# Row maxima by single chunk and bank, one copy of sums and values per head, and a division on gathered sums

## The reference

```python
q_pool = q.reshape(B, H, S // 2, 2, D).mean(axis=3)          # S = 1152, D = 64: 576 query rows
scores = (1 / sqrt(D)) * np.matmul(q_pool, k.transpose(0, 1, 3, 2))   # 576 x 1152
scores = scores - np.max(scores, axis=-1, keepdims=True)
attn = np.exp(scores)
attn = attn / (np.sum(attn, axis=-1, keepdims=True) + 1e-09)
x = np.matmul(attn, v)                                        # 576 x 64 of each head
h = x @ w_in;  x = (h * tanh(softplus(h))) @ w_out            # 1152 tokens, 512 -> 2048 -> 512
h = x @ w_in2; x = where(h > 0, h, exp(min(h, 0)) - 1) @ w_out2
```

## Time and profile before

| | |
|---|---|
| time, median of 3 runs | 705.26 us (703.49 to 706.42) |
| the profiled execution | 703.71 us, its span 701.9 us |
| PE busy, share of the span | 657.8 us, 94% |
| POOL, DVE, ACT busy | 426.5, 423.4, 397.0 us |
| waits of PE for the reduction of maxima | 14.9 us in 32 waits |

### The profile page before, as it was taken

The page is one execution under the profiler, slowest core; times in us unless marked ns, Lnnn a source line. Parts: engine busy times, 40 slices in busy tenths (PEclk is TensorE's granted clock), DMA queues, the critical chain, the costliest instruction groups (busy, mean ns, idle before and its releaser), DMA issues.

```text
span 701.9 us, 12236 instructions
## 1 busy us (share of the span) xinstructions
PE 657.8 (94%) x3984; PEld 636.7 (91%) x3984; DVE 423.4 (60%) x620; ACT 397.0 (57%) x743; POOL 426.5 (61%) x388
## 2 busy tenths in 40 slices
PE   3589999999999999999999999999999999999997
PEld 2478889898898988899999999999999999999997
DVE  6667878787887876377777665777543332223222
ACT  2357888888888878755555555555643322222221
POOL 4266788888888866587786666787644422222221
PEclk9599999999999999999999999999999999999999
DMA  5355564555556540012220000122222110001001
GB/s 162 96 155 157 147 174 135 163 159 158 143 147 163 157 110 16 16 50 71 62 61 0 0 0 30 48 67 67 60 77 61 46 45 0 0 0 46 1 1 45
DMA packets 31503, 54.30 MB, mean 77 GB/s; under 512 B 4752, under 2 KB 10208, under 8 KB 31456
## 3 DMA queue, kind: packets, MB, share of 16 engines
q1 hardware_dynamic: 31296, 53.66, 27.7%
q10 hardware_dynamic: 160, 0.04, 0.0%
HBM read 30.93 MB, written 2.36 MB: 47 GB/s over the span
## 4 chain that ended last, share of the span: by engine, by line
PE 67%; POOL 8%; ACT 8%; DVE 7%; issue 7%; DMA 2%; SPq 1%; POOLq 0%; ACTq 0%; DVEq 0%
PE py L490 9%; PE py L491 8%; PE py L492 8%; PE pH L475 8%; PE pH L476 8%; PE pH L477 8%; PE pm L398 5%; DVE part_max L712 3%; PE po L430 3%; PE po L431 3%; PE po L432 3%; PE ps L413 3%; PE ps L414 3%; POOL pl L931 3%; ACT ph L565 2%
## 5 line engine op out<-in xcount | busy, mean ns | idle before, releaser
L986 POOL TENSOR_TENSOR gl<-fg,gh 128x384 fp32r<-128x384 f32 x96 | 97.3, 1014 | 142.4 <-ACT gh L655 141.1
L931 POOL TENSOR_TENSOR pl<-p,ph 128x576 fp32r<-128x576 f32 x72 | 106.0, 1480 | 67.4 <-ACT p L571 63.3
L712 DVE TENSOR_REDUCE part_max<-pm 128x2 f32<-128x768 f32 (+1 forms) x123 | 111.1, 904 | 39.9 <-PE pm L398 38.1
L490 PE MATMUL py<-gh,wout_h 128*128 128x384 f32 x384 | 129.2, 336 | 3.6 <-DVE xl L842 2.2
L491 PE MATMUL py<-gl,wout_h 128*128 128x384 f32 x384 | 128.4, 334 | 0.0
L492 PE MATMUL py<-gh,wout_l 128*128 128x384 f32 x384 | 128.3, 334 | 0.0
L477 PE MATMUL pH<-xh,win_l 128*128 (+1 forms) x384 | 128.3, 334 | 0.0
L475 PE MATMUL pH<-xh,win_h 128*128 (+1 forms) x384 | 128.3, 334 | 0.0
L476 PE MATMUL pH<-xl,win_h 128*128 (+1 forms) x384 | 128.3, 334 | 0.0
L565 ACT ACTIVATE ph<-ps 128x576 fp32r<-128x576 f32 x144 | 93.9, 652 | 51.2 <-PE ps L414 48.8
L821 DVE RECIPROCAL fi<-fp 128x192 f32<-128x192 f32 x48 | 64.9, 1353 | 52.2 <-POOL fp L994 52.1
(11 more groups left out here) (68 smaller groups left out, 1367.7 us busy)
## 6 DMA issues: line engine op xcount, KB each, us to landing
kh<-k_hi SPq DMA_DIRECT2D x60, 144.0 KB, 2.6
w_raw<-w_in SPq DMA_DIRECT2D x32, 256.0 KB, 2.7
w_raw<-w_out SPq DMA_DIRECT2D x32, 256.0 KB, 2.6
k_pack<-kP SPq DMA_DIRECT2D x16, 288.0 KB, 3.2
q_raw<-qT SPq DMA_DIRECT2D x16, 288.0 KB, 3.1
v_raw<-v SPq DMA_DIRECT2D x16, 288.0 KB, 2.9
kl<-k_pack SPq DMA_DIRECT2D x32, 144.0 KB, 2.4
q<-q SPq DMA_DIRECT2D x16, 144.0 KB, 2.5
```

The source lines that it names most:

```text
L490: pe.matmul(out, hi, gh[:, f % 4, :], start=(f == 0), stop=False)
L712: dve.tensor_reduce(part_max[:, par, 2 * g:2 * g + wide], group_banks(n, g)[:, 0:wide, 0:MC], AX.X, ALU.max).then_inc(m_read, 1)
L931: pool.tensor_tensor(pl[:, ph_slot(slot, kt), :], p32[:, p32_slot(n, kt) % 3, :], ph[:, ph_slot(slot, kt), :].bitcast(F32), ALU.subtract). ...
```

## The change

1. **Maxima.** From head 1 on, a chunk of 384 columns goes to one of the banks `pm` alone, and is reduced alone: 15 reductions a head in place of 8, and PE fills one bank while DVE reads the other. Head 0 keeps its groups. Four chunks of head 1 come before the first scores.
2. **Copy.** One copy a head of all 128 rows of `po` into `o_rows`, at the first step of the next head instead of two copies of 64 rows at the last step.
3. **Division.** `gather_sums` moves a row of 576 sums of each head to 64 x 9 elements; DVE adds 1e-9 and inverts 128 x 9; `gather_inv` brings each half back as one row of `inv_wide`, and `spread_inv` copies that row to 63 partitions; `move_o` brings the odd head's values to the lower partitions; `finalize` is one multiplication. `scale_by_partner`, `multiply_sums`, `copy_sum` are gone. These transfers are all issued on SP's queue, as `spread_row` now is too.
4. **Order.** `pv` always follows the scores of its step; `POOL_KT` alternates; the splits of k, q, v, w and x move to other steps; DVE's stream is written by chunk. SP's order is new.

```diff
-POOL_KT = ((2, 4, 5, 6, 8), (2, 4, 5, 8))
+POOL_KT = ((1, 3, 5, 7, 8), (1, 3, 5, 7))
...
-FIRST_GROUPS = (2, 2, 2, 2, 0, 1, 1, 1, 2)
-GROUPS = (1, 1, 1, 0, 1, 1, 1, 1, 1)
-
-
-GPSIMD_AT = {"split_v": (0, 0), "multiply_sums": (1, None), "sum_q": (3, 3), "split_w": (4, 4),
-             "split_k": (6, 6), "split_q": (7, 7), "split_x": (None, 7)}
-SCALAR_AT = {"split_v": (0, 0), "split_w": (2, 2), "spread_row": (4, 4), "round_k": (4, 4), "split_q": (5, 5),
-             "split_x": (None, 5)}
-VECTOR_AT = {"scale": (1, None), "invert_0": (3, None), "invert_1": (5, None), "finalize": (None, 3)}
+
+EARLY_CHUNKS = 4
+FIRST_CHUNKS = ((2, 1), (2, 1), (2, 2), (1, 0), (1, 1), (1, 1), (1, 1), (1, 1), (1, 1))
+CHUNKS = ((1, 0), (2, 0), (2, 0), (0, 0), (2, 0), (1, 1), (2, 0), (1, 1), (1, 1))
+
+
+FIRST_SPLIT_BEHIND = {3: (1, 0), 6: (1, 2), 10: (1, 4), 14: (1, 6)}
+SPLIT_BEHIND = {3: (2, 8), 5: (1, 0), 8: (1, 2), 12: (1, 4), 14: (1, 6)}
+INVERT_BEHIND, FINALIZE_BEHIND = 14, 6
+
+
+GPSIMD_AT = {'split_k': (0, 0), 'sum_q': (3, 2), 'split_v': (3, 1), 'split_q': (8, 4), 'split_w': (5, 7), 'split_x': (0, None)}
+SCALAR_AT = {'split_v': (0, 0), 'split_w': (1, 2), 'round_k': (3, 5), 'split_q': (7, 6), 'split_x': (None, 7)}
...
+            def gather_sums(m):
+                par, pair = m % 2, m // 2
+                sp.wait_ge(o_copied, m + 1)
+                wait(sp, sum_kept, pair)
+                source = D * (1 - par)
+                sp.dma_start(sum_few[par * D:par * D + D, :],
+                             o_rows[source:source + 1, par, :].rearrange("o (r c) -> o r c", c=FEW)).then_inc(sums_in[par], 16)
+
+            def move_o(p):
+                sp.wait_ge(o_copied, 2 * (p + 1))
+                sp.wait_ge(sums_in[0], 16 * (p + 1))
+                sp.dma_start(o_rows[D:2 * D, 0, :], o_rows[D:2 * D, 1, :]).then_inc(o_moved, 16)
+
+            def gather_inv(p):
+                sp.wait_ge(sum_inv, p + 1)
+                wait(sp, x_ready, p)
+                for par in range(2):
+                    sp.dma_start(inv_wide[par * D:par * D + 1, :].rearrange("o (r c) -> o r c", c=FEW),
+                                 inv_few[par * D:par * D + D, :]).then_inc(inv_in, 16)
+
+            def spread_inv(p):
+                sp.wait_ge(inv_in, 32 * (p + 1))
+                for par in range(2):
+                    first = par * D
+                    sp.dma_start(inv_wide[first + 1:first + D, :],
+                                 inv_wide[first:first + 1, :].unsqueeze(1).to_broadcast([1, D - 1, SQ])).then_inc(inv_spread, 16)
...
             next_q(1)
             spread_kl(0)
             spread_q2(0)
+            spread_row(0)
             next_q(2)
             spread_kh(1)
             spread_q1(1)
...
             for n in range(HEADS):
-                if n + 2 < HEADS:
-                    load_v(n + 2)
                 if n + 1 < HEADS:
                     load_w(w_in[0][n + 1], 0, n + 1, (n + 1) % 2)
+                if n % 2 == 0 and n > 0:
+                    gather_sums(n - 1)
+                    move_o(n // 2 - 1)
+                elif n % 2:
+                    gather_sums(n - 1)
+                if n + 1 < HEADS:
+                    spread_row(n + 1)
+                if n % 2 == 0 and n > 0:
+                    gather_inv(n // 2 - 1)
                 if n + 2 < HEADS:
                     spread_kl(n + 2)
                     spread_q2(n + 2)
+                if n % 2 == 0 and n > 0:
+                    spread_inv(n // 2 - 1)
+                if n + 2 < HEADS:
+                    load_v(n + 2)
                 if n + 3 < HEADS:
                     spread_kh(n + 3)
                     spread_q1(n + 3)
                 if n + 4 < HEADS:
                     next_q(n + 4)
                     load_kp(n + 4)
+            gather_sums(HEADS - 1)
+            move_o(PAIRS - 1)
+            gather_inv(PAIRS - 1)
+            spread_inv(PAIRS - 1)
...
+            def max_chunk(n, j):
+
+                at, (t, c) = chunk_count(n, j), divmod(j, 3)
+                if j == 0:
                     pe.wait_ge(kh_spread, 64 * (n + 1))
                     pe.wait_ge(q1_spread, 64 * (n + 1))
-                wait(pe, m_read, NG * n + g - (2 if n == 0 else 0))
-                for j in range(2 * g, min(2 * g + 2, NCH)):
-                    t, c = divmod(j, 3)
-                    mm = pe.matmul(group_banks(n, g)[:, j % 2, 0:MC], q1[:, n % 3, t * P:t * P + P],
-                                   kh[n % 3][:, c * MC:c * MC + MC], start=True, stop=True)
-                mm.then_inc(m_filled, 1)
+                wait(pe, m_read, at - 1)
+                pe.matmul(pm[:, at % 2, 0:MC], q1[:, n % 3, t * P:t * P + P], kh[n % 3][:, c * MC:c * MC + MC],
+                          start=True, stop=True).then_inc(m_filled, 1)
...
+            for j in range(EARLY_CHUNKS):
+                max_chunk(1, j)
...
                     nxt = ahead(n, kt)
-                    if kt + AHEAD < KT:
+                    if nxt is not None:
                         scores(*nxt)
-                        for head, g in groups_at(n, kt):
-                            max_group(head, g)
-                        pv(n, kt)
-                    else:
-                        pv(n, kt)
-                        if nxt is not None:
-                            scores(*nxt)
-                        for head, g in groups_at(n, kt):
-                            max_group(head, g)
+                    for head, j in chunks_at(n, kt, 0):
+                        max_chunk(head, j)
+                    pv(n, kt)
+                    for head, j in chunks_at(n, kt, 1):
+                        max_chunk(head, j)
...
-                wait(act, x_scaled, n // 2)
-                own = slice(n % 2 * D, n % 2 * D + D)
-                act.activation(halves(o_pair[own, :]), po[own, :, 0:HQ], ACT.Copy).then_inc(o_copied, 1)
-
-            def copy_sum(n):
-
-                wait(act, sum_prod, n // 2)
-                own, other = slice(n % 2 * D, n % 2 * D + D), slice(D - n % 2 * D, 2 * D - n % 2 * D)
-                act.activation(halves(sum_pair[own, :]), po[other, :, 0:HQ], ACT.Copy, bias=1e-9).then_inc(sum_copied, 1)
+                if n % 2 == 0:
+                    wait(act, x_ready, n // 2)
+                else:
+                    wait(act, o_moved, 16 * (n // 2))
+                    wait(act, sums_in[1], 16 * (n // 2))
+                act.activation(halves(o_rows[:, n % 2, :]), po[:, :, 0:HQ], ACT.Copy).then_inc(o_copied, 1)
...
+            def max_chunk(n, j):
+                at, par = chunk_count(n, j), n % 2
+                dve.wait_ge(m_filled, at + 1)
+                dve.tensor_reduce(part_max[:, par, j:j + 1], pm[:, at % 2, 0:MC], AX.X, ALU.max).then_inc(m_read, 1)
+                if j == NCH - 1:
+                    dve.wait_ge(m_read, at + 1)
+                    turn_row(n)
...
+            def invert(p):
+
+                dve.wait_ge(sums_in[0], 16 * (p + 1))
+                dve.wait_ge(sums_in[1], 16 * (p + 1))
+                dve.tensor_scalar(sum_few[:, :], sum_few[:, :], 1e-9, None, ALU.add).then_inc(sum_kept, 1)
+                dve.wait_ge(sum_kept, p + 1)
+                wait(dve, inv_in, 32 * p)
+                dve.reciprocal(inv_few[:, :], sum_few[:, :]).then_inc(sum_inv, 1)
...
+            def finalize(p):
+                dve.wait_ge(inv_spread, 32 * (p + 1))
+                dve.wait_ge(o_moved, 16 * (p + 1))
                 wait(dve, xl_done, p)
-                dve.tensor_tensor(halves(x_pair[:, :]), halves(o_pair[:, :]), halves(sum_pair[:, :])[:, ::-1, :],
-                                  ALU.mult).then_inc(x_scaled, 1)
-
-            def finalize(p):
-                dve.wait_ge(sum_inv, 2 * (p + 1))
-                dve.wait_ge(x_scaled, p + 1)
-                dve.tensor_tensor(halves(x_pair[:, :]), halves(x_pair[:, :]),
-                                  inv_pair[:, :].unsqueeze(1).to_broadcast([P, 2, HQ]),
-                                  ALU.mult).then_inc(x_ready, 1)
+                dve.tensor_tensor(x_pair[:, :], o_rows[:, 0, :], inv_wide[:, :], ALU.mult).then_inc(x_ready, 1)
...
+            for m in range(1, HEADS + 2):
+                for j in range(NCH):
+                    if m < HEADS:
+                        max_chunk(m, j)
+                    if j == INVERT_BEHIND and m % 2 and 3 <= m < HEADS:
+                        invert((m - 3) // 2)
+                    if j == FINALIZE_BEHIND and m % 2 == 0 and 4 <= m <= HEADS:
+                        finalize((m - 4) // 2)
+                    if j in (SPLIT_BEHIND if m > 1 else FIRST_SPLIT_BEHIND):
+                        back, kt = (SPLIT_BEHIND if m > 1 else FIRST_SPLIT_BEHIND)[j]
+                        if 0 <= m - back < HEADS and kt in VKT[(m - back) % 2]:
+                            split_p(m - back, kt)
+
+            invert(PAIRS - 1)
```

(62 more changed lines are left out.)

105 lines of the change are left out of this document (51 added, 54 removed).

## The result

| | before | after |
|---|---|---|
| time, median | 705.15 us (703.49 to 706.42) | 775.37 us (773.92 to 776.05) |
| the profiled execution | 703.71 us, span 701.9 | 776.05 us, span 774.1 |
| mean granted clock of PE | 0.987 | 0.933 |

What follows compares the result with a forecast made beforehand. PE was taken as the bound, with a gap of about a tenth in attention. Pairs -13.0, start +2.3, end of attention -1, into the network +6.6 sum to -5.1: 700.2 us against the median of 705.26, range 690 to 709.

Steps and rivals of the forecast that it cites:

- Its landing is the unknown ... I take 3.0: Division: spread_inv lands 3.0 us after its last issue begins, so PE loses 1.0 us a pair with the restart.
- The broadcast lands late: Division, rival at 0.20: both spread_inv read one partition and land at 3.9 us instead of 3.0; 705 us.
- the count of engines: Division: by the Trainium skill's rule the broadcast's 63 partitions go to 9 DMA engines, making the late landing likelier.
- What the clock took: Start of the network: PE's clock falls in a 5.8 us gap and costs +2 us (0 to +5.8).
- The chunks: Maxima in attention: PE's 2.35 us a pair of waits for the reduction go, if DVE is not held.
- One copy and splits: Attention pairs: the single copy costs 0.3 us in one head of two; 0.23 us a pair stays for splits.
- The start: Head 0: moves queued behind spread_row delay first scores to about 30.3 us; step 5 comes +2.3 us (0 to +5).
- The end of attention: Last heads: no chunks, alternating tiles, the last one DVE's; -1 us (-2 to +1).
- Into the network: From attention to the first network: the division's transfers and finalize delay multiply_h by 4.6 us, +6.6 with the clock.
- The SP rival: SP's queue, rival at 0.17: 39 issues a pair become the bound, from 0.73 us an issue; 712 us.
- Seven pairs: Attention, step 5 of head 0 to head 14: 1.85 us less a pair, -13.0 us in all.

Runs made afterwards that it cites:

- the mended kernel: Changed kernel with the inverse through HBM, start, end and SP order moved, no 1e-9 addition, last product one chunk earlier: 690.22 us, ratio 0.9797.

## Why the prediction was wrong

**The step that failed** is one number: "Its landing is the unknown ... I take 3.0". What leads up to it came out within a microsecond. Counted from step 0 of the even head, where the prediction's t begins (its scores start at 110.41 in the pair shown), the last scores of the head began at 8.8 (8.2 counted), `spread_kl` was issued at 9.7 (8.9), the last `spread_inv` at 12.3 (11.3), and DVE stood ready for `finalize` at 13.9 (13.15). The inverse was to be there at 14.3 and came at 23.1. The landing was not 3.0 but 10.8 us. With that number alone the prediction's own sum gives a stall of 0.9 + 7.8 = 8.7 a pair; measured 8.6 here, and 8.5 in the mean of six pairs.

**Why 3.0 was taken.** Of the rows that it lay between the earlier trace rows one reads 64 partitions and the other HBM (`k_pack<-kP`); the broadcast reads one partition. The text said so ("no row shows such a read"), and yet bounded the unknown by 2.0 and 3.9. That was no bound from rows, since none of them showed the case. A range without an upper row had to be left open upward, and the forecast with it, since the order of SP's queue puts DVE and PE behind this landing.

**The rival that named the place** was priced wrong. "The broadcast lands late" had the mechanism, one source partition, and put its size at 0.9 us, for which it showed no row. The runs part it from the count of engines, the rule that stood beside it: 63 rows instead of 64 cost 1.8 us where each row has its own partition and at most 0.6 where all come from one; the single partition costs 7.8 (11.0 against 3.2). In the Trainium skill, "SBUF — State Buffer", section "Door 1: The DMA port swizzle (why `[64,N]` ≈ `[32,N]`)", four neighbouring partitions share one port of about 27 GB/s. An estimate by that page for one transfer of 145 KB is 5.4 us of reading. The run has 8.6 us for one transfer alone, 1.8 of which is the median landing of `gather_inv`'s 2.2 KB: 6.8 for the rest, and the page is borne out in kind. By that estimate a landing is 7.2 us, 4.2 later than taken, in seven pairs and at the end: a rival at about 734.

**What the clock took.** It was counted at the end (+2) but not in a pair, since a gap of 1 us was forecast there. The gap of 8.2 to 8.6 brought it down in each of the six pairs, and with it 2.1 us in the mean. So a pair of 41.3 instead of 30.55 is, roughly, 7.5 us of longer stall, 2.1 of clock, 0.8 of the splits below, and 0.4 of `invert`'s wait. Only six of the seven pairs have a division beside them; the sum took the stall for all seven.

**The chunks.** "The 2.35 us go, if DVE is not held" held only in the new order: with chunks alone 0.1 of it came in six pairs. In the mended kernel the profile shows no idle time of PE ahead of `pm` in pairs of 30.4. So the term is right in the whole, and wrong as a part.

**One copy and splits** were under-sized together, and mistaken in kind. 0.3 + 0.23 a pair were counted. In a mended pair of 30.4 the first `pv` of each head starts 0.45 us late, but what ends that wait is DVE's split of tile 0 (done at 82.71, PE at 82.74); the copy was done at 82.48, so it cost nothing by itself. The other 0.2 in each head stand behind the two chunks in a row at step 6, where the second waits for its bank. That is 1.3 in all:

```profile
82.74 0.37 PE L496 MATMUL po<-ph,vt 128*128 128x288 f32 x1 [0.21 <-DVE pl L790]
```

That is why a pair without any stall is 30.4 (30.41 measured; 29.0 + 1.3 is 30.3) and not 29.5.

**Two terms were left out.** `invert` can wait for its gathered sums, ahead of a split: up to 1.5 us a pair. The sums' 2.2 KB were taken to land in 2.1 us; in the changed kernel they took 3.3 in the median and 4.3 at most. And DVE's small operations were taken at the length of work without a neighbour, 0.4 for addition and inversion together and 0.8 for the product; beside GpSimd the addition took up to 1.46 and the product up to 1.98.

**The start** was right in kind: first scores at 29.95 (30.3 counted), step 5 of head 0 at +0.9 instead of +2.3, inside its bounds. **The end of attention** was to gain 1; it lost 7.8, since the copy of head 14 waits for the product of the pair before, and PE for that copy (8.3). **Into the network** the chain was counted right but for the same landing: from the first issue of `gather_inv` to that of `spread_inv` 3.1 us (2.7 counted), then 11.1 to `finalize` instead of 3.3:

```profile
356.79 1.16 SPq L370 DMA_DIRECT2D inv_wide<-inv_few  x2
359.93 1.60 SPq L377 DMA_DIRECT2D inv_wide<-inv_wide  x2
```

```profile
370.99 0.76 DVE L806 TENSOR_TENSOR x_pair<-o_rows,inv_wide 128x576 f32<-128x576 f32 x1 [14.23 <-DMA inv_wide<-inv_wide]
```

**The SP rival** (712) did not come: 1.59 us for two issues of the broadcast, 0.8 each, but the queue's lateness followed the broadcast and wasn't its cause, since without it the pair is 31.2 with all other issues in place.

**Slips of the sums**, none of which moves the forecast: by the earlier trace rows DVE's reductions before come to 13.1 us a pair, not 13.4; the case of the late broadcast adds up to +2.1, not +2.3; and at the start the clock came back 11.6 us after PE resumed, not 11.7.

**The rest of the idea was sound.** Seven pairs were to gain 13.0 us; in the mended kernel (690.22 us) they gain 11.75 (215.7 against 227.5), the start 1.5, the end of attention 1.3, the way into the network 0.4, and the network loses 0.4: 14.5 of span.

## What to carry to other kernels

Before a transfer is priced by its bytes, ask from how many partitions it reads and by what its row count divides: here the time out of one source partition grew with the rows, and a row in HBM, or a source of 64 partitions, brought 11 us down to 3 to 5. An unknown that stands ahead of other work in an in-order queue is not one term of a sum; it can grow without cover, so measure it first or put what waits for it last. And when a wait is removed, ask which engine has no gap around that place: with chunks alone the gain stayed out, by my reading (no run shows it) for ACT's and POOL's backlog.

## What the runs showed of the hardware

- Two transfers, each from one partition, are not independent: one alone 8.6 us, two from partitions 0 and 64 11.0, two from the same one 12.8. In the Trainium skill, "SBUF — State Buffer", section "Door 1: The DMA port swizzle (why `[64,N]` ≈ `[32,N]`)", partitions 0 and 64 lie on different ports; what they share here stays open.
- 61 rows of 2304 bytes, each from its own partition, two transfers: 16.1 us; 64 rows: 3.2.
- DVE's addition on 128 x 9 elements took 0.17 to 1.46 us and its product of two SBUF tensors 0.76 to 1.98, by what GpSimd was doing; its reciprocal of one tensor (0.20 to 0.22) and its splits, which read PSUM (0.71 to 0.76), kept their length. The Trainium skill, "SBUF — State Buffer", section "🔬 SBUF: two separate sides", has an exclusive lock of the port pair that a DVE operation with two SBUF inputs, or in a 2-port mode, shares with GpSimd; the trace agrees, with 110.80 and 204.90 as the two orders.
- In the six long gaps of the changed kernel the granted clock fell to the 1.2 GHz level 2.1 to 4.3 us after PE stopped, and rose 3.7 to 6.0 us after it started again; at the start of the kernel before the rise took 11.6 us, with waits in between the earlier trace rows.
- While the broadcasts held the DMA engines, single issues on SP's queue took up to 3.6 us (288 KB, `v_raw`) and 4.4 us (144 KB, `kh`), against 0.6 for each of four in a row before.
